# Channel attention and FFN on one core: eight row chunks scored as three fp32r products, with the weight loads and roundings rearranged around them

## The reference, cut to what matters

```python
B, N, C = 2, 6016, 256                 # q, k, v: float32; w_in [256, 2048], w_out [2048, 256]
qn = q / (norm(q, axis=1) + 1e-6)      # norms over the 6016 rows, one per channel
kn = k / (norm(k, axis=1) + 1e-6)
s = kn.transpose(0, 2, 1) @ qn / tau   # [B, 256, 256]: a sum over 6016 rows
a = softmax(s)
x = (v @ a).reshape(B * N, C)
h = x @ w_in
out = (h * sigmoid(h)) @ w_out         # silu between the two products
```

## Time and profile before

| | us |
|---|---|
| median of 3 runs | 1080.24 (1080.08 to 1080.40) |
| the profiled execution's own time | 1081.3 |
| its span, first to last instruction | 1078.6 |
| PE busy | 1073.3 (100%) |
| DVE / ACT / POOL busy | 724.2 / 622.8 / 35.6 |

### The profile page before, as it was taken

How to read it: one execution, slowest core, us unless ns; L and a number is a source line. 1 busy time by engine, 2 the same in 40 slices (tenths; PEclk the granted TensorE clock), 3 DMA queues, 4 the chain that set the end, 5 groups by cost and what they waited for, 6 DMA issues and landing times.

```text
span 1078.6 us, 12990 instructions
## 1 busy us (share of the span) xinstructions
PE 1073.3 (100%) x4824; PEld 906.3 (84%) x4824; DVE 724.2 (67%) x943; ACT 622.8 (58%) x782; POOL 35.6 (3%) x24
## 2 busy tenths in 40 slices
PE   9999999999999999999999999999999999999998
PEld 8888888888888888888899888888888888888998
DVE  6778588567567566566688777566566566566665
ACT  6787665565555555554666555555555555555654
POOL 2460000000000000000000000000000000000000
PEclk9999999999999999999999999999999999999999
DMA  9990000200200200200200200200200200200100
GB/s 340 393 401 18 1 1 1 78 1 1 79 1 1 78 0 0 73 0 0 79 1 1 74 1 1 79 1 1 79 1 1 78 0 0 73 0 0 40 1 34
DMA packets 26140, 54.06 MB, mean 50 GB/s; under 512 B 2544, under 2 KB 7408, under 8 KB 26096
## 3 DMA queue, kind: packets, MB, share of 16 engines
q1 hardware_dynamic: 25376, 52.60, 13.3%
q10 hardware_dynamic: 720, 0.89, 0.2%
HBM read 41.16 MB, written 12.32 MB: 50 GB/s over the span
## 4 chain that ended last, share of the span: by engine, by line
PE 97%; DMA 2%; SPq 0%; DVE 0%; ACT 0%; issue 0%; ACTq 0%
PE ps_o L423 16%; PE ps_o L424 16%; PE ps_o L425 16%; PE ps_h L389 14%; PE ps_h L390 14%; PE ps_h L388 14%; PE ps_o L351 6%; DMA qk<-k_dram 2%; PE ps_o L382 0%; PE ps_o L380 0%; PE ps_o L381 0%; SPq L258 0%; DVE q_scale L733 0%; PE ps_h L380 0%; PE ps_h L382 0%
## 5 line engine op out<-in xcount | busy, mean ns | idle before, releaser
L390 PE MATMUL ps_h<-b_hi,a_lo_rest 128*128 128x512 f32 (+1 forms) x504 | 194.1, 385 | 0.0
L389 PE MATMUL ps_h<-b_lo,a_hi_rest 128*128 128x512 f32 (+1 forms) x504 | 194.1, 385 | 0.0
L388 PE MATMUL ps_h<-b_hi,a_hi_rest 128*128 128x512 f32 (+1 forms) x504 | 194.0, 385 | 0.0
L839 DVE TENSOR_TENSOR h_b<-ps_h,u 128x512 f32<-128x512 f32 x96 | 66.4, 692 | 166.6 <-PE ps_h L390 166.5
L820 DVE TENSOR_TENSOR u<-ps_h,u 128x512 f32<-128x512 f32 x96 | 66.4, 691 | 142.3 <-PE ps_h L390 91.0
L625 ACT ACTIVATE h_a<-ps_h 128x512 f32<-128x512 f32 x96 | 57.4, 598 | 162.1 <-PE ps_h L390 162.1
L424 PE MATMUL ps_o<-g_lo_a,wo_hi 128*128 128x512 f32 (+1 forms) x384 | 147.9, 385 | 0.0
L423 PE MATMUL ps_o<-g_hi_b,wo_hi 128*128 128x512 f32 (+1 forms) x384 | 147.9, 385 | 0.0
L425 PE MATMUL ps_o<-g_hi_b,wo_lo 128*128 128x512 f32 (+1 forms) x384 | 147.9, 385 | 0.0
L423 PE MATMUL ps_o<-g_hi_a,wo_hi 128*128 128x512 f32 (+1 forms) x384 | 147.9, 385 | 0.0
L424 PE MATMUL ps_o<-g_lo_b,wo_hi 128*128 128x512 f32 (+1 forms) x384 | 147.8, 385 | 0.0
(11 more groups left out here) (120 smaller groups left out, 1537.7 us busy)
## 6 DMA issues: line engine op xcount, KB each, us to landing
v_raw<-v_t_dram SPq DMA_DIRECT2D x40, 256.0 KB, 3.6
out_t_dram<-v_raw SPq DMA_DIRECT2D x20, 512.0 KB, 3.2
qk<-q_dram SPq DMA_DIRECT2D x15, 384.0 KB, 10.4
qk<-k_dram SPq DMA_DIRECT2D x15, 384.0 KB, 12.1
wp_raw<-q_dram SPq DMA_DIRECT2D x8, 384.0 KB, 10.7
wp_raw<-k_dram SPq DMA_DIRECT2D x8, 384.0 KB, 11.7
home<-q_dram SPq DMA_DIRECT2D x6, 384.0 KB, 10.2
home<-k_dram SPq DMA_DIRECT2D x6, 384.0 KB, 10.9
```

What stands on the lines that cost most here:

```text
L388: nc.tensor.matmul(ps_h[:, bank, 0:n], w_hi, x_hi, start=start, stop=False, skip_group_check=True)
L389: nc.tensor.matmul(ps_h[:, bank, 0:n], w_hi, x_lo, start=False, stop=False, skip_group_check=True)
L390: return nc.tensor.matmul(ps_h[:, bank, 0:n], w_lo, x_hi, start=False, stop=stop, skip_group_check=True)
```

## The change

- `SPLIT = (5, 8, 11, 14, 20, 24, 27, 30)`: these eight 3-row chunks are scored as three fp32r products. After squaring such a chunk ACT rounds all of it, 128x1536, into `qk_parts` (`round_rows`); POOL subtracts (`split_rows`); PE multiplies (`score_parts`), 18 matmuls of 128x256. There are two such buffers (`SETS`). PE takes a split chunk later than its number says (`LAG`): it runs 0-4, 6, 7, 5, 9, 10, 8, 12, 13, 11, 15, 16, 17, 14, 18, 19, 21, 22, 23, 20, 25, 26, 24, 28, 29, 27, 31, 32, 33, 30. The ring slot of a split chunk is free once POOL has split it.
- w_in has a buffer of its own. It is loaded with chunks 8, 11, 14, 17, and POOL both rounds and subtracts it.
- w_out is loaded behind the last chunk. ACT rounds two quarters of it before the first `copy_folded` and two in pair 0 of the opening step; DVE subtracts all four there, in place.
- ACT issues the key loads of 7 chunks instead of 4.
- The DVE and ACT jobs for batch 0's softmax and v's first tile are spread over more chunks.
- One more `copy_folded` of batch 0 stands ahead of ACT's exponentials of batch 1.

The diff, cut to its core:

```diff
-KEYS_BY_ACT = 4
+KEYS_BY_ACT = 7
+SPLIT = (5, 8, 11, 14, 20, 24, 27, 30)
+LAG = 3
+SETS = 2
...
+    ORDER = sorted(range(len(CHUNKS)), key=lambda g: (g + LAG, 1) if g in SPLIT else (g, 0))
+    PLACE = [ORDER.index(g) for g in range(len(CHUNKS))]
...
                 if g >= RING:
-                    sp.wait_ge(chunk_scored, g - RING + 1)
+                    if g - RING in SPLIT:
+                        sp.wait_ge(rows_split, SPLIT.index(g - RING) + 1)
+                    else:
+                        sp.wait_ge(chunk_scored, PLACE[g - RING] + 1)
                     sp.wait_ge(chunk_squared, 2 * (g - RING + 1))
...
-                if g in (7, 10, 13, 16):
+                if g in (8, 11, 14, 17):
+                    n = (g - 8) // 3
+                    sp.dma_start(w_in_part(w_in_raw, n), w_in_parts[n // 2, n % 2]).then_inc(w_in_loaded[n], 16)
...
-                if g in (20, 22, 24, 26):
...
+            for n in range(PARTS):
+                sp.dma_start(wo_raw[:, n * FK // PARTS:(n + 1) * FK // PARTS, :], w_out_parts[n]).then_inc(
+                    wo_loaded[n], 16)
...
+            def split_rows(n):
+                pool.wait_ge(rows_rounded, n + 1)
+                parts = [qk_parts[n % SETS][:, i].rearrange("p i r c -> p (i r c)") for i in range(2)]
+                nc.gpsimd.tensor_tensor(parts[1], qk[SPLIT[n] % RING][:, :, :, :].rearrange("p i r c -> p (i r c)"),
+                                        parts[0].bitcast(F32), ALU.subtract).then_inc(rows_split, 1)
+
+            def round_and_split_w_in(n):
+                pool.wait_ge(w_in_loaded[n], 16)
+                nc.gpsimd.tensor_copy(w_in_part(w_in_hi, n), w_in_part(w_in_raw, n)).then_inc(w_in_rounded, 1)
+                pool.wait_ge(w_in_rounded, n + 1)
+                nc.gpsimd.tensor_tensor(w_in_part(w_in_lo, n), w_in_part(w_in_raw, n),
+                                        w_in_part(w_in_hi, n).bitcast(F32), ALU.subtract).then_inc(w_in_split, 1)
...
+            def score_parts(g):
+                b = CHUNKS[g][0]
+                n = SPLIT.index(g)
+                pe.wait_ge(rows_split, n + 1)
+                hi, lo = (qk_parts[n % SETS][:, i] for i in range(2))
+                for r in range(ROWS):
+                    for c in range(CK):
+                        out, d = ps_s[b][:, c * C:(c + 1) * C], slice(c * P, (c + 1) * P)
+                        nc.tensor.matmul(out, hi[:, 1, r, d], hi[:, 0, r, :], start=False, stop=False,
+                                         skip_group_check=True)
+                        nc.tensor.matmul(out, hi[:, 1, r, d], lo[:, 0, r, :], start=False, stop=False,
+                                         skip_group_check=True)
+                        mm = nc.tensor.matmul(out, lo[:, 1, r, d], hi[:, 0, r, :], start=False, stop=False,
+                                              skip_group_check=True)
                 mm.then_inc(chunk_scored, 1)
...
+            def round_rows(g):
+                n = SPLIT.index(g)
+                if n >= SETS:
+                    act.wait_ge(chunk_scored, PLACE[SPLIT[n - SETS]] + 1)
+                nc.scalar.activation(qk_parts[n % SETS][:, 0], qk[g % RING][:, :, :, :], ACT.Copy).then_inc(rows_rounded, 1)
...
+            def split_wo(n):
+
+                dve.wait_ge(wo_rounded, n + 1)
+                nc.vector.tensor_tensor(wo_part(wo_lo, n), wo_part(wo_raw, n), wo_part(wo_hi, n).bitcast(F32),
+                                        ALU.subtract).then_inc(wo_split, 1)
```

More of the change, by code:

```diff
@@ L55, in channel_attention_ffn @@
     SECOND = ENDS[0]
+    ORDER = sorted(range(len(CHUNKS)), key=lambda g: (g + LAG, 1) if g in SPLIT else (g, 0))
+    PLACE = [ORDER.index(g) for g in range(len(CHUNKS))]
+    assert all(CHUNKS[g][2] == ROWS and g + LAG < len(CHUNKS) and CHUNKS[g][0] == CHUNKS[g + LAG][0] for g in SPLIT)
     WIDE = N // (2 * TOK)
@@ L92, in channel_attention_ffn @@
         a_lo_first = sb("a_lo_first", [P, EARLY, FACTORS, P], F32R)
+        with ExitStack() as early:
+            qk_parts += [sb("qk_parts1", [P, 2, 2, ROWS, C], F32R, stack=early)]
         wp_raw += [sb("wp_raw1", [P, PAIRS, 4, P])]
@@ L107, in channel_attention_ffn @@
             w_in_hi = sb("w_in_hi", [P, CK, F], F32R, stack=early)
+            with ExitStack() as first:
+                w_in_raw = sb("w_in_raw", [P, CK, F], stack=first)
             w_in_lo = sb("w_in_lo", [P, CK, F], F32R, stack=early)
@@ L161, in channel_attention_ffn @@
         chunk_added = sem("chunk_added")
+        rows_rounded = sem("rows_rounded")
+        rows_split = sem("rows_split")
         rows_added = sem("rows_added")
@@ L313, in _ @@
             nc.gpsimd.memset(square_sum[1][:], 0.0).then_inc(sums_cleared, 1)
[L315 to L318, removed]
+            def split_rows(n):
[9 more added lines that the diff above has]
+                                        w_in_part(w_in_hi, n).bitcast(F32), ALU.subtract).then_inc(w_in_split, 1)
+            split_rows(0)
+            for n in range(PARTS - 1):
+                split_rows(n + 1)
+                round_and_split_w_in(n)
+            round_and_split_w_in(PARTS - 1)
             pool.wait_ge(v_loaded, 64)
@@ L336, in _ @@
                                     b_hi[0][:, T3:T4 + 1, :].bitcast(F32), ALU.subtract).then_inc(v_split, 1)
[L338 to L341, removed]
+            for n in range(6, len(SPLIT)):
+                split_rows(n)
         @block.tensor
@@ L479, in _ @@
                 nc.tensor.matmul(ps_turn[:, 0:P], ones[:], ones[:], start=True, stop=True)
-            for g in range(len(CHUNKS)):
-                score_chunk(g)
+            for g in ORDER:
+                if g in SPLIT:
+                    score_parts(g)
+                else:
+                    score_chunk(g)
                 if g == SECOND + 1:
@@ L608, in step @@
                     if opening and pair == 0:
+                        for part in range(PARTS // 2, PARTS):
+                            round_wo(part)
+                        act.wait_ge(chunk_scored, len(CHUNKS))
                         for group in range(FOLDS // 2):
@@ L658, in _ @@
                 if g == SECOND + 5:
+                    round_t12(0, 0)
+                if g == SECOND + 7:
+                    round_t34(0, 0)
+                if g == SECOND + 8:
                     exponentials(0)
-                    round_t34(0, 0)
-                if g in (25, 26, 27, 28):
-                    round_w_in(g - 25)
                 if g == SECOND + 13:
                     round_probs(0)
+            for n in range(PARTS // 2):
+                round_wo(n)
             copy_folded(0, 0)
@@ L668, in _ @@
             nc.scalar.activation(scratch[:], ones[:, 0:1], ACT.Exp)
-            for group in range(1, 3):
+            for group in range(1, 4):
                 copy_folded(0, group)
@@ L672, in _ @@
             round_a(0, 0)
-            for group in range(3, FOLDS - 1):
+            for group in range(4, FOLDS - 1):
                 copy_folded(0, group)
@@ L828, in step @@
                         c22_made, 1)
-                    if not (opening and pair == 0):
+                    if opening and pair == 0:
+                        for part in range(PARTS):
+                            split_wo(part)
+                    else:
                         split_b(n - 1)
```

37 lines of the change are left out of this document (18 added, 19 removed).

## The result

The changed kernel took 1084.25 us (median of six runs, 1083.69 to 1084.83), the kernel before 1079.88 on the same chip. The ratio is 1.004 with a 95% interval of 1.0027 to 1.0053: slower, by more than 0.2%. The profiled execution took 1084.13 us, 1082.3 of it span. The forecast was 1081.4 (case A, within 0.2%). The range of 1077.6 to 1085.2 held the time, but what happened is rival B, priced at 1084; the time lies in the range because the range was stretched to B.

A forecast was written before the change was run, and what follows sets the result against it. PE was taken as the bound, loads nearly tied. Matmuls -3.5, key waits +1.75, loads -0.9, handovers +1.6 and +2.35, fold -0.3 came to +1.0, by the walk +1.2: 1081.4 us, range 1077.6 to 1085.2.

The forecast's parts named there:

- case A: At the handovers of chunks 24 and 27, two waits of about 2 us each eat the gain: 1081.4 us, chance 0.44.
- rival B: At DVE's small k_scale steps, POOL holds DVE more than once, making chunk 23's adds late: 1084 us, chance 0.27.
- rival E: In the split chunks, three passes of 256 columns cost what 512 do: about +9.7 us, 1091, chance 0.03.
- Term 3: Two handovers of split chunks through ACT and POOL: PE waits 1.6 us before chunk 24 and 2.35 before 27.
- Term 1: Scoring matmuls on PE: a split chunk takes 2.16 us, 0.44 less for each of eight, 3.5 in all.
- Term 2: Loads ahead of chunk 19: 0.9 us shorter, starting it at 48.3; the first four split chunks' savings become key waits.
- Rival C: At the handovers from chunk 20 to 27, none is late: faster, 1077.4 us, chance 0.16.
- Rival D: POOL's rounding copy of w_in costs 2.35 us instead of 1.0: about +2, 1083.4 us, chance 0.10.
- Term 4: Behind the scores: folds from 90.9 us, 1.5 later; the extra copy removes a 0.31 us wait; w_out work costs nothing.

The follow-up runs named there:

- b_later: The changed kernel with a_psum's edit, chunks 24 and 27 scored behind 28 and 32, probabilities turned one chunk later: 1077.64 us against 1080.0, ratio 0.9975.
- a_nosplit: The changed kernel with no split chunk, all 34 chunks scored in fp32: 1079.72 us against 1080.38 for the kernel before, ratio 0.9994.
- a_psum: The changed kernel with the three small DVE steps on q_scale and k_scale reading PSUM instead of SBUF: 1080.9 us against 1080.38, ratio 1.0003.
- a_warm: The changed kernel with eleven unused fp32 matmuls on PE ahead of chunk 24's wait: 1084.78 us against 1080.38 for the kernel before, ratio 1.0036.
- c_before_psum: The kernel before with the three small DVE steps reading PSUM: 1080.28 us against 1080.0, ratio 1.0001.
- b_pool_sub: The kernel before with two more POOL subtractions of 512 elements behind the 1024 one: 1083.95 us in a single execution.
- b_pool_set: The kernel before with one more POOL memset of 1024 elements behind the 1024-element subtraction: 1081.28 us in a single execution.
- a_t12late: The changed kernel with v's 1024-element POOL subtraction moved behind the split of chunk 24: 1082.33 us against 1079.91 for the kernel before, ratio 1.0021.

## Where the prediction was right and where it was wrong, step by step

The range held the time, and that was luck as far as the forecast goes: its upper end was there for B and E. The forecast itself, case A, put the change at 1.2 us slower, and it measured 4.4. One step of its walk failed, the small DVE work on k_scale (Term 3).

**Term 1 held.** Within a split chunk matmuls follow each other every 0.12 us. Start to start a split chunk shows 2.34 us, but the fp32 chunk ahead of it shows 2.40 instead of 2.59 (67.44 to 69.84 in b_later): the switch of format moves the border between the two, not the sum. Together 4.74, less 2.59, is 2.15 for the split chunk; 2.16 was forecast. Nothing of rival E was seen. Reading 2.34 alone would book 0.25 us of saving for 0.43.

**Term 2 held in its sum, by luck.** The forecast put chunk 19 at 48.3, 0.9 earlier, and 51.77 for 52.66 is that 0.9. But it booked all of it to earlier loads and nothing to the first four split chunks. Without split chunks the earlier loads are worth 0.07 us (52.59 in a_nosplit); what there is comes from the split chunks, PE waits for keys at chunk 6 and not at 19, and 0.9 was the best of five executions, of which one gained nothing (52.84 in a_psum).

**Term 3 failed, at one step of the walk.** PE's readiness for 24 was forecast at 67.0 and is 67.0; the waits are at 24 and 27 and at no other split chunk, as forecast. What failed is "0.7 us of small work on k_scale". The forecast had those steps end at 61.05; they end at 63.79, as L790, L791 and L792 together take 3.8 us from 60.01 on. The 2.75 us of delay run on unchanged: POOL hands chunk 24 over at 71.4, where 68.6 was forecast, and chunk 27 at 81.56 for 78.75. I had the evidence in the earlier trace rows, where the q_scale step was held, and applied it to that one step, because no row showed a k_scale step beside POOL. There was none to see: in the kernel before, POOL had a gap until its next job by then. The rows of an undisturbed step said nothing about the disturbed one. The rest of the walk was near: it had 39.1 us from the first chunk behind the norms to the first fold, with 0.7 us of hold on q_scale in it, and a_psum, without any hold, shows 38.07.

The wait at 27 was forecast as 2.35 us and is 0.55 here, mainly since the clock made PE 1.65 us late for it. The forecast had no lower clock in it. By a_warm and a_psum (1.72 and 2.07 with the clock at 1.00) the size of that step was about right.

**Rival B was right in mechanism and in price.** It had chunk 23's adds at 64.45 and the time at 1084.8 if both k_scale steps were held; the adds came at 63.82, the time at 1084.25. The Trainium skill (VectorE: DVE Perf Modes, "Mode 2×_2P — use both read ports for one tensor") asks, for the mode that uses both ports, for operands in SBUF and an even outermost dimension, which two elements meet. The traces agree that such steps are held: 1.29 and 2.26 us from SBUF beside POOL, 0.16 and 0.22 from PSUM beside POOL (c_before_psum). Rival B deserved more than 0.27, for nothing in the row that spoke for the hold depended on the size of the operand.

**Rival C** was shown possible, but only with other handovers (b_later), not by this change. **Rival D** is refuted by the line of the copy, by form (count, busy us, mean ns):

```profile
L344 POOL CAST w_in_hi<-w_in_raw 128x1024 fp32r<-128x1024 f32 x4 | 4.2, 1050 | 0.0
```

1.05 us, where 1.0 was taken.

**Term 4 held, and was worth more.** The wait of 0.31 at the folds is gone: from the first fold to the first product it takes 12.33 us, before 12.96. That is 0.6 where 0.3 was forecast. w_out's new place shows no wait in the opening pair. The folds come at 93.78 instead of 90.9 through Term 3 alone.

## What to carry to other kernels

- If a trace shows one instruction stretched until another engine's instruction ends, every later instruction of that kind is a candidate, however small; walk it against the other engine's new schedule before summing. Three such steps here, 0.7 us of work, took 3.8 us more.
- Work handed through two engines needs a lead longer than the whole path, the waits of those engines on third parties included. Handovers in series refill each other: closing the wait at 24 opened 2.07 us at 27, and a higher clock mostly lengthened the next wait.
- A border between two kinds of matmul is read over both neighbours, not on one side.

## What the runs showed of the hardware that was not expected

- A POOL memset, which reads nothing, holds a DVE tensor_scalar as a subtraction does (0.95 us of memset inside a step of 2.20).
- Reciprocals are not held: L935 and L791 took 0.15 and 0.17 us, the first beside a POOL subtraction. Nor are tensor_scalar steps with a PSUM source: 0.42, 0.16 and 0.22 us under one POOL subtraction in c_before_psum.
- Whether a waiting step gets in between two POOL instructions back to back differed: yes between the subtractions (b_pool_sub), no between subtraction and memset (b_pool_set). One run each; the reason is open.
- In the changed kernel the clock fell to the lower level 0.9 us after PE had resumed from its 4.33 us of idling, and PE was busy all the while until it came back: the granted clock is 0.50 from 73 to 75 us, 0.58 from 75 to 76 and 1.00 from 76 on.
- A DVE tensor_tensor with both inputs in SBUF and a POOL instruction that reads SBUF hold each other. The changed kernel has two such adds beside POOL, which were alone before, at 0.69 us each: the first takes 1.29 us now, the second 2.77. DVE, then POOL:

```profile
44.50 2.77 DVE L785 TENSOR_TENSOR square_sum<-square_sum 128x512 f32<-128x512 f32 x1
44.00 2.72 POOL L346 TENSOR_TENSOR w_in_lo<-w_in_raw,w_in_hi 128x1024 fp32r<-128x1024 f32 x1
46.69 1.72 POOL L356 TENSOR_TENSOR t_raw<-v_raw 128x512 f32<-128x512 f32 x1
```

  The second add ends 0.55 us behind POOL's 1024-element subtraction, and POOL's own instructions grow as well, from 2.36 to 2.72 us and from 1.27 to 1.72. The forecast's walk began behind this place. ACT waited 3.72 us for DVE here; in a_t12late and a_psum it waited 3.6 us there for keys anyway, so no cost at the folds is shown. Together with the steps above it means that the engines of this kernel meet at more than semaphores.
